# Two small constant tiles change their place in the on-chip memory of a gated attention and feed-forward kernel

## The reference

```python
# 1. recurrent gated attention: batch 2, 8 heads, 768 steps, 40 channels
m_new = np.maximum(f_gate[:, :, t] + m, i_gate[:, :, t])
C = f_stab * C + i_stab * np.einsum('bhd,bhe->bhde', vt, kt)
n = f_stab * n + i_stab * kt
h_tilde = C @ qt;  denom = max(|n . qt|, 1)
y[:, :, t] = sigmoid(o_gate[:, :, t]) * h_tilde / denom
# 2. 1536 tokens x 320 channels
xn = x / sqrt(mean(x * x) + 1e-6) * rms_g
x = (silu(xn @ w_gate) * (xn @ w_val)) @ w_out        # 320 -> 1536 -> 320
# 3.
h = x @ w_in;  out = maximum(0.01 * h, h) @ w_out2    # 320 -> 2048 -> 320
```

## Time and profile before

| | us |
|---|---|
| median of 3 runs | 474.05 (473.7 to 474.48) |
| the profiled execution, its own time | 473.7 |
| its span, first to last instruction | 471.9 |

### The profile page before, as it was taken

One profiled execution on the slowest core, in us unless ns is written; L12 is line 12 of the kernel. 1 busy time (PEld: TensorE's weight loads), 2 busy tenths in 40 slices (PEclk: granted clock), 3 DMA queues, 4 the chain that ended last, 5 costly groups with the idle time before them and its releaser, 6 DMA issues.

```text
span 471.9 us, 7144 instructions
## 1 busy us (share of the span) xinstructions
PE 449.8 (95%) x2722; PEld 417.7 (89%) x2722; DVE 264.7 (56%) x492; ACT 179.9 (38%) x350; POOL 105.6 (22%) x95
## 2 busy tenths in 40 slices
PE   3769899999999999999999999999999999999997
PEld 3769898999999999999988888889989989998996
DVE  7657768676666786765553343634333343453444
ACT  1564552524233343242433322655334343333332
POOL 3488748312213031100042210253000000000000
PEclk9789999999999999999999999999999999999999
DMA  5968452403122131300022200230000000010101
GB/s 155 291 215 260 160 184 77 117 15 104 47 71 83 36 119 36 129 1 0 2 61 78 76 31 1 58 96 0 1 0 1 1 1 0 1 56 1 57 0 56
DMA packets 21439, 31.64 MB, mean 67 GB/s; under 512 B 1328, under 2 KB 15296, under 8 KB 21408
## 3 DMA queue, kind: packets, MB, share of 16 engines
q1 hardware_dynamic: 21408, 31.22, 21.1%
HBM read 29.20 MB, written 2.02 MB: 66 GB/s over the span
## 4 chain that ended last, share of the span: by engine, by line
PE 81%; DVE 8%; issue 4%; ACT 3%; DMA 2%; POOL 1%; SPq 0%; DVEq 0%; POOLq 0%; ACTq 0%
PE gate_ps L947 21%; PE value_ps L947 21%; PE out_ps L1013 8%; PE out_ps L976 8%; PE even_ps L1013 3%; PE odd_ps L1013 3%; PE c_ps L1013 3%; PE out_ps L980 3%; PE odd_ps L922 2%; PE c_ps L900 2%; PE odd_ps L891 2%; PE even_ps L891 2%; DMA att_sb<-in_qk 1%; PE c_ps L911 1%; DVE h_lo L766 1%
## 5 line engine op out<-in xcount | busy, mean ns | idle before, releaser
L766 DVE TENSOR_TENSOR h_lo<-hid,h_hi 128x512 fp32r<-128x512 f32 (+2 forms) x96 | 74.6, 777 | 62.1 <-ACT h_hi L502 62.1
L502 ACT ACTIVATE h_hi<-hid 128x512 fp32r<-128x512 f32 (+2 forms) x96 | 55.5, 579 | 127.5 <-DVE hid L753 89.2
L947 PE MATMUL gate_ps<-x_hi,w_sb 128*128 128x512 f32 (+2 forms) x288 | 69.6, 363 | 3.6 <-DVE act_buf L747 2.6
L947 PE MATMUL value_ps<-x_hi,w_sb 128*128 128x512 f32 (+2 forms) x288 | 69.2, 362 | 0.0
L947 PEld LDWEIGHTS gate_ps<-x_hi,w_sb 128*128 128x128 f32 x288 | 48.6, 189 | 9.1 <-issue 3.2
L947 PEld LDWEIGHTS value_ps<-x_hi,w_sb 128*128 128x128 f32 x288 | 49.3, 191 | 4.2
L490 ACT ACTIVATE act_buf<-gate_ps 128x384 f32<-128x384 f32 (+2 forms) x48 | 23.4, 488 | 69.2 <-PE gate_ps L947 69.1
L976 PE MATMUL out_ps<-h_hi,w_sb 128*128 128x384 f32 (+2 forms) x192 | 48.5, 336 | 0.5 <-DVE h_lo L766 0.5
L747 DVE SCALAR_TENSOR_TENSOR act_buf<-act_buf,gate_ps 128x384 f32<-128x384 f32 (+2 forms) x48 | 26.5, 551 | 35.5 <-ACT act_buf L490 35.4
L392 POOL TENSOR_TENSOR w_sb<-raw,w_sb 128x704 fp32r<-128x704 f32 x16 | 27.5, 1717 | 75.3 <-ACT w_sb L484 75.3
L1013 PE MATMUL out_ps<-w_sb,h_hi 128*128 128x320 f32 x192 | 42.9, 308 | 0.0
(11 more groups left out here) (164 smaller groups left out, 809.5 us busy)
## 6 DMA issues: line engine op xcount, KB each, us to landing
raw<-in_w SPq DMA_DIRECT2D x12, 544.0 KB, 5.2
att_sb<-in_tok SPq DMA_DIRECT2D x12, 512.0 KB, 4.7
expo<-decay_scratch SPq DMA_DIRECT2D x12, 512.0 KB, 5.9
raw<-in_w SPq DMA_DIRECT2D x16, 352.0 KB, 2.9
att_sb<-in_qk SPq DMA_DIRECT2D x24, 160.0 KB
out_y<-y_acc SPq DMA_DIRECT2D x12, 160.0 KB, 1.9
consts_sb<-in_consts SPq DMA_DIRECT2D x1, 129.5 KB, 2.3
gates_sb<-in_gates SPq DMA_DIRECT2D x1, 96.0 KB, 2.4
```

The costliest lines, as they stand in the source:

```text
L502: nc.scalar.activation(h_hi[:, r, 0:n], hid[:, r, 0:n], ACT.Copy).then_inc(hi_done, 1)
L766: nc.vector.tensor_tensor(h_lo[:, r, 0:n], hid[:, r, 0:n], h_hi[:, r, 0:n].bitcast(F32), ALU.subtract).then_inc(h_done, 1)
L947: last = nc.tensor.matmul(ps[:, 0:n], lhs, rhs, start=(j == 0), stop=(j == len(xs) - 1))
```

## The change

Two of the allocation calls are written further down: `consts_sb` and `minus_half` are now taken after `raw` instead of ahead of `x_hi`. No instruction is added, removed or put elsewhere: on all five engines the instructions of the two programs stand in the same order, with the same operands by name and shape and the same waits.

```diff
@@ -103,17 +103,15 @@
             return stack.enter_context(nc.sbuf_tensor(name, shape, dt))
 
 
-        consts_sb = sb(ctx, "consts_sb", [P, 2 * P + KT])
-        minus_half = sb(ctx, "minus_half", [P, 1])
         x_hi = sb(ctx, "x_hi", [P, 2, TILES * P], F32R)
         x_lo = sb(ctx, "x_lo", [P, 2, TILES * P], F32R)
         x_odd = sb(ctx, "x_odd", [P, TILES * P], F32R)
         raw = sb(ctx, "raw", [P, RAW, W1RAW])
-
+        consts_sb = sb(ctx, "consts_sb", [P, 2 * P + KT])
         ident_sb = consts_sb[:, 0:P]
         last_row_sb = consts_sb[:, P:2 * P]
         rms_sb = consts_sb[:, 2 * P:]
-
+        minus_half = sb(ctx, "minus_half", [P, 1])
         tail = sb(ctx, "tail", [HP, CHUNK])
```

## The result

The changed kernel takes 476.49 us in the median (475.98 to 477.69, six runs); the kernel before, run beside it, 473.61 (472.88 to 474.48, six runs). The ratio is 1.0064, with a 95% interval of 1.0050 to 1.0079: **slower by about 2.9 us**, above the range of the prediction and on the side to which it had given 8%. That is small, but the interval leaves out 1: the kernel before never took longer than 474.48 us in these runs, and the kernel after never less than 475.98.

The account below looks back on a forecast made before the run. It took PE's matmul count times their distance to bound the kernel from 45 us on, with engine waits before; terms of 0 + 0 + 0 + 0 left 473.7 us for the profiled execution, median forecast 474.0 us, range 473.0 to 475.2.

Parts of the forecast that it names:

- the side to which it had given 8%: Whole kernel slower by over 0.2%, the 8% of two or more new POOL and DVE collisions.
- What bounds the kernel: From 45 us on, a count of matmuls times the distance between them; ahead of that, waits between engines.
- PE streaming x: 1152 matmuls streaming x tiles, whose starts go from 64 to 0 modulo 128; taken as 0, bound 3.5 us either side.
- the pair L900 and L922: Plain float32 matmuls on state and att_sb, different starts, both median 275 ns; taken to show a start costs 0.
- the accesses to those six: Cost as a sum over accesses to the six tiles whose first byte differs, each times a possible difference.
- The evenness of the earlier trace: Four streamed tiles at different places, all 64 modulo 128, show about 13 ns extra per matmul; distance between tiles doesn't matter.
- the 3 ns between L932 and L891: Identity transpose at 272 ns against att_sb product at 275; bounds the start's effect at -3 to +3 ns per 128 columns.
- a start at a multiple of 128 makes streaming cheaper: Rival, matmuls on x: 3 ns each gives 470.5 us, all 13 ns gives 459.0 us; chance 8%.
- collisions: Rival, DVE subtractions falling on POOL's ahead of 110 us: one hit 474.8 us, two 475.6; two or more 8%.
- The other terms: ACT and DVE on x and raw, the constants, and transfers into raw: each taken as 0.
- The 256-byte rule for transfers: Transfers into raw: 140 beats instead of 142, 1.4% less, 0.05 us per slice; 1.3 us if on the path, taken 0.
- The sign posts in the prediction: If streaming is right: 0.227 us between x_hi matmuls, 3.60 us per layer 3 step, 836 matmuls in 150 us.

Follow-up runs that it names:

- e2: x and raw exactly where the changed kernel has them, everything behind raw (weights, h included) 64 bytes lower; 473.59 us beside 474.33, ratio 0.9989.
- e9: Kernel before with w2_sb1, the weights of layer 3's second half, 64 bytes higher, y_acc behind it; one execution, 473.74 us beside 472.52.
- e1: Close to the changed kernel, but x tiles 64 bytes higher and last_row_sb split from consts_sb; 474.0 us beside 474.33, ratio 1.0009.
- e8: x at distance 0 from the weights as in the kernel before, h_hi and h_lo 64 bytes lower; ratio 1.0016.
- e6: All x tiles 64 bytes above the weights' start, where the changed kernel has them 64 below; 475.89 us beside 473.97, ratio 1.0073.
- e12: Kernel before, layer 3 given its own h tiles 64 bytes below the weights' start modulo 256; one execution, 473.69 us beside 472.52.
- e11: Kernel before, layer 3 given its own h tiles 128 bytes from the weights' start modulo 256; one execution, 475.12 us beside 472.52.

## Why the prediction was wrong

**What bounds the kernel** was read rightly: from chunk 1 on the time is the number of matmuls times the distance between them, and that is where the 2.9 us came. The prediction also named the right accesses, PE streaming x, as the one term that could matter, and the right place to look.

**The step that failed is the size of that term, set to 0 from the pair L900 and L922.** It measured 2.6 us on x, and 0.6 us more on h. The pair are plain float32 matmuls. The earlier trace rows hold the warning: 96 columns (L900, L922) and 128 columns (L891) show the same 275 ns, and their starts follow each other every 112 ns with either count. An operation whose time doesn't follow its column count isn't bound by its streaming, so it can't show what slows streaming. In the kernel after the medians are 275 ns again.

The pair was also misread. The prediction has L900 read `state` at every 656 bytes from a start at 0 modulo 128. The kernel steps by `2 * DV`, 82 columns or 328 bytes, and the second of the two buffers lies 1696 bytes behind the first. So only one of its eight starts is at 0 modulo 128, and L900 is hardly a row of "a start at 0". The right neighbours would have been other fp32r matmuls, and of these the trace had none at another distance. That should have been put down as "not shown", with the bound kept on both sides.

**The sum left out what did not move.** The prediction summed over "the accesses to those six" tiles. h isn't among them, and its matmuls lost 0.21 us in chunk 3, 0.23 and 0.15 in the chunks with 384 columns: a matmul inherits something from the stream ahead of it.

**The evenness of the earlier trace rows was misread.** x and h gave the same 227 ns at four places, and the prediction concluded that only the value modulo 128 was left untested. It listed the starts of the streamed tiles but never set them against the start of what is loaded meanwhile. The table in the section on the change had both, though only modulo 128. All four tiles, and the weights in both layers, shared one value modulo 256 (192); that was the condition under which 227 ns held. e2 and e9 show that the distance, and not the value, decides.

**The bound came near by luck, and its upper side was dropped.** From the 3 ns between L932 and L891 the prediction had up to 3.5 us on either side for 1152 matmuls, and the loss is 2.9. But the 3 ns came from plain float32 matmuls of 128 columns, a transpose against a product, and were carried to 256 to 512 columns of fp32r unchanged. The matmuls on x lost 6.2, 2.3, 1.9 or 0.9 ns each, by stage. In any case only the lower side was made a rival (a start at a multiple of 128 makes streaming cheaper, 8%); for slower, only collisions were kept. The time moved the other way (233 ns against 227 with 512 columns). Only with 256 columns did it fall (114 against 120), where it is worth nothing, and by e2 the multiple of 128 has no part in either.

**The other terms held.** ACT's copies out of `raw` and POOL's subtractions are where they were in the earlier trace rows, within 7 ns in the median:

```profile
L482 ACT ACTIVATE w_sb<-raw x28: 772/778/1117, 18.1 to 325.0; 128x704 fp32r<-128x704 f32 x16, 128x1088 fp32r<-128x1088 f32 x12
L390 POOL TENSOR_TENSOR w_sb<-raw,w_sb x16: 1700/1707/1803, 235.9 to 325.9; 128x704 fp32r<-128x704 f32 x16
```

e1 and e2 take `raw` and the constants out of the question with 1.0009 and 0.9989. The 256-byte rule for transfers, which the prediction quotes from the Trainium skill, brought nothing that shows: its 1.4% would be 0.05 us per landing, and the median landing was 3.3 us before, 3.6 after and 3.4 in e2, where `raw` starts as it does after. **Collisions** between POOL and DVE didn't decide either: L766 (now L764) has a longest duration of 2480 ns after and 2489 before, and the stretch from the first matmul on x to chunk 1, where they would cost, takes 59.1 us in both.

**The sign posts in the prediction worked.** It said that a failed streaming term would be seen in the distance between 512-column matmuls on `x_hi` (0.227 us) and in the step of layer 3, and that is where it was seen: 0.233 us in chunk 3, and 3.607 us instead of 3.593 for the step. The count of 836 matmuls in 150 us fell to 834.

What stays open: why the distance matters at all, that is, what the two reads share, and why 64 bytes cost with 512 columns, pay with 256, do nothing that shows with 320 and, from the two chunks with 384, cost 0.3 to 0.6 us per chunk. That the second read is the weight load was not shown by taking the loads away; it rests on e2, e8 and e9, in which moving the loaded tile or the streamed tile has the same effect.

The Trainium skill says on its page TensorE: Matmul & The Clock Gate, section Step-by-step: what each phase is for, that TensorE streams and loads weights through two independent read ports, and that the load takes nothing from the running matmul's reads. By that rule the place of the loaded tile shouldn't change what streaming costs. With x at the same bytes the kernel after shows 233 ns and e2 227, by where the weights are, and e9 shows 1.84 and 1.87 us for the same eight matmuls. The trace doesn't agree for fp32r operands, and the measurement decides.

## What to carry to other kernels

An edit that only moves tiles in the on-chip memory can change TensorE's speed. In a kernel bound by matmuls, write down the start of each streamed tile and of each loaded one modulo 256 before and after, and keep their distance if it is 0. Read the distance between the starts of successive matmuls rather than their durations or PE's busy share, and compare it with the column count; a few ns there, times a thousand, is the whole effect. Before you take a row as a neighbour, see whether its time follows what you are about to vary. And when a trace shows the same number everywhere, look for what all those places have in common before calling the number insensitive.

## What the runs showed of the hardware that was not expected

- In the last chunk of layer 2, fp32r matmuls of 512 columns follow each other every 227 ns where streamed and loaded tile start at the same value modulo 256, and every 233 ns at a distance of -64 bytes; +64 gives 230 on average (3.68 us for 16), 128 and, in a mixed run, small distances of 8 to 16 bytes 233 to 234 (3.73 and 3.74 us for 16). In layer 3, behind matmuls of 320 columns, the same ones average 230 ns at distance 0 and 232 at -64 (1.838 and 1.856 us for 8).
- With 256 columns it is the other way round: 120 ns at distance 0, 114 at +64 (e6) and at -64 (the kernel after). With 320, twelve take 1.755 us at 0, 1.753 at -64 (e8, e12) and 1.765 at 128 (e11).
- The distance counts and the place does not: all tiles 64 bytes off, together, give back 64.96 us for twelve steps, to the hundredth.
- Passing from matmuls with one distance to matmuls with another costs about 20 ns spread over the next five (e8: 226, 236, 228, 233, 231 ns, then 227). Passing from 320-column matmuls that stream weights to 512-column ones that stream x does the same at one distance (before, layer 3: 231, 236, 228, 233, 231 ns, then 226 to 227).
